# Block-sparse attention with a gated MLP on one core: q and k transposed by the whole array, and a new order of every queue

## The chip, the cores and the metric

The kernel runs on one core of a Trainium2 chip. The time is device time in microseconds (us) of one execution, the median over the runs shown. Five engines work side by side, each through its own queue in order: TensorE (PE; its weight loads are PEld), VectorE (DVE), ScalarE (ACT), GpSimd (POOL) and SyncE (SP), which here does nothing but issue DMAs.

## The reference

The input is q, k, v of shape (4 batches, 8 heads, 768 tokens, 64) and the weights of a gated MLP. Attention is causal and block-sparse: for each token the 6 best of 24 chunks of 32 keys are kept. A chunk's rank is an upper bound of the score, from the minimum and maximum of its keys.

```python
k_min = np.min(k_chunks, axis=3); k_max = np.max(k_chunks, axis=3)
ub = np.sum(np.maximum(q[..., None, :] * k_min[:, :, None], q[..., None, :] * k_max[:, :, None]), axis=-1)
ub = np.where(causal, ub, -1e9)
top_chunks = np.argsort(ub, axis=-1)[..., -6:]
scores = np.where(sel & causal_tokens, scale * q @ k.T, -1e9)
x = softmax(scores) @ v            # heads side by side: (batch, 768, 512)
h = gelu(x @ w_in); u, v = h[..., :512], h[..., 512:]
v_n = (v - mean) / sqrt(var + 1e-6) * g_ln
out = x + (u * (w_sg @ v_n + b_sg)) @ w_out
```

## The kernel before

**Work.** Two heads make a pair; there are 16 pairs, p = 0 to 15, four to a batch. For a pair, q and k come from memory token by token (128 tokens on the partitions, 6 groups of tokens, the two heads' 64 numbers side by side, tile `qn` or `kn`), are transposed on PE by `transposed`, lines 581 to 587 (matmul against the identity `identF`, line 567), and copied out of PSUM: q into `qT` (line 659), k of pairs 0 to 5 into `KA` (line 606), with the chunks' minimum and maximum taken from the same PSUM banks (line 596). For pairs 6 to 15 k is transposed by a DMA (line 623) and its minima come from line 613, so PE transposes 6 k's and 16 q's, 22 in all. The chunk bounds are the small matmuls of lines 696 (pairs 0 to 3) and 743; DVE picks the best six and makes a mask; scores are the matmuls of lines 852 and 858 (pairs 0 to 3, each head on 64 rows of the array) and 812 (pairs 4 to 15, the whole array); ACT takes the exponential (lines 873, 818); the product with v is lines 896 and 903, and line 919 scales it into `XS`.

**Transposing, as it is.** `tokens_T` (lines 561 to 570) issues 12 matmuls: for each of the 6 groups of tokens, the first 64 tokens on the upper half of the array's rows into one PSUM bank and the last 64 on the lower half into another (`tile_position=(64 * R, 0)`). The program counts the change between such row tiles and the whole array as a change of mode. Both banks are written by one entry of PE's queue, so both are given out at once, and bank R holds runs of 64 tokens that `half` (line 575) spreads over `qT` or `KA`.

**The MLP of a batch.** When the four pairs of a batch are in `XS`, it is transposed into `xT` (line 935 on PE for batch 0 and part of 3, otherwise by DMA, line 927). Then `moe_h`: six matmul groups for v (line 950), gelu (line 954), statistics (lines 959, 961, 963), the reciprocal root on POOL (line 965), its use (line 967), and the normalised `vhat` (line 978 on DVE, 973 on ACT); eight groups for u (line 990). `moe_g`: eight groups against w_sg (line 1007), each of which needs all of `vhat`; lines 1013 and 1017 on DVE; then the output product (line 1030), the residual into `osb` (line 1036, three buffers in turn), and the store (line 1043).

**Order.** All operations of the whole program are made once, as a list, and `TABLE` holds for each engine the numbers of that list in the order of its queue, the PSUM bank of each tile (`slots`) and the engine of those operations that can run on more than one (`engine`). Dependencies become semaphore waits by themselves; every queue is strictly in the order of its row. Five stages can be told apart on PE: start to batch 0's first line 950 (pairs 0 to 3), then from each batch's first line 950 to the next (attention of the next four pairs mixed with the MLP of this batch), and the last batch's MLP alone.

Of the kernel before, what the change touches and what calls it, by code (L numbers as in the profile page):

```python
# [249 lines left out]
def pe32(*cols):  # L250
    o = sum(c * 2 / 2.4 + 2.5 for c in cols) + 28
    return o, o + 136
# [6 lines left out]
def _build(nc, ctx, q, k, v, w_in, g_ln, w_sg, b_sg, w_out, out):  # L259
# [4 lines left out]
    NT = S // 128  # L264
    NC = S // 32
# [50 lines left out]
    RUN2 = 0  # L316
    FINE = (0,)
# [254 lines left out]
    def run(p):  # L572
        return 128 if p < RUN2 else 64

    def half(a, R, p):
        return a.rearrange("p (a R x) -> p R a x", R=2, x=run(p))[:, R]
# [4 lines left out]
    def transposed(p, nm, src, tag):  # L581
        s = p % NQS
        ts = [ps_g.tile() for _ in range(2)]
        P.op("pe", (pairs_T if p < RUN2 else tokens_T)(src[s], ts), (650, 820) if p < RUN2 else (412, 580), (tag, p),
             mode=3 if p < RUN2 else 1,
             reads=[(nm, s, i, h) for i in range(2) for h in range(2)] + ["identF"] + ["pewarm"] * (p == 0), writes=ts, alloc=tuple(ts))
        return ts

    def kside(p):
        w = p % NW  # L590
        ts = transposed(p, "kn", kn, "ktr")
        wv = lambda R, m: W[w][:, m, 0:NC].rearrange("p (a R c) -> p R a c", R=2, c=run(p) // 32)[:, R]
# [519 lines left out]
    for p in range(4, NP + 4):  # L1112
# [38 lines left out]
    "act": (  # L1151
# [10 lines left out]
    "dve": (  # L1162
# [105 lines left out]
```

How the kernel before makes its waits and increments, by code:

```python
        def run(e, eng):  # L186
            for i in self.order[e]:
                o = ops[i]
                need = {}
                for d in o.waits:
                    p = ops[d]
                    s = dsem[p.dma] if p.dma is not None else sems[p.eng]
                    key = p.dma if p.dma is not None else p.eng
                    if key not in need or need[key][1] < p.count:
                        need[key] = (s, p.count)
                for s, c in need.values():
                    eng.wait_ge(s, c)
                ins = o.fn(eng)
                if o.dma is not None:
                    ins.then_inc(dsem[o.dma], 16)
                elif o.inc:
                    ins.then_inc(sems[e], 1)
            if e == "sp":
                for d, idxs in self.dma_sems.items():
                    if ops[idxs[-1]].tag[0] == "st":
                        eng.wait_ge(dsem[d], 16 * len(idxs))
```

## Time and profile before

| | us |
|---|---|
| median of 3 runs | 216.65 |
| lowest, highest | 216.13, 218.79 |
| the profiled execution's own time | 217.55 |
| its span, first to last instruction | 215.4 |

The span lies inside the own time; 2.15 us lie around it. Times in rows count from the start of the span. Rows of a timeline give start, duration, engine, line, operation, what is written from what, shapes and count; in brackets the idle time of the engine just before and what ended it. A matmul's row includes its way through the array, so a matmul that follows at once starts before the row of the one ahead has ended; how long a group holds PE is read from its start to the start of the next.

### The profile page before, as it was taken

How to read it: one execution, taken by the hardware profiler on the slowest of the kernel's cores; microseconds unless marked ns; L12 is line 12 of the kernel's file. 1: busy time of each engine (PE TensorE's matmuls, PEld its weight loads, DVE VectorE, ACT ScalarE, POOL GpSimd, SP SyncE). 2: the span in 40 equal slices, each digit the busy share in tenths (PEclk: the TensorE clock that was granted, in tenths of full speed). 3: DMA queues.
4: the chain of work that ended last, by engine and by line, in shares of the span. 5: the costliest groups of instructions: out<-in, count | busy, mean ns of one | idle time of the engine just before them, and what ended most of it. 6: DMA issues, size and time to landing. Idle time of an engine off the chain costs nothing.

```text
span 215.4 us, 6383 instructions
## 1 busy us (share of the span) xinstructions
PE 194.8 (90%) x2549; PEld 126.0 (58%) x2564; DVE 185.5 (86%) x531; ACT 163.7 (76%) x247; POOL 132.8 (62%) x168
## 2 busy tenths in 40 slices
PE   7778897899999999997959989998995999999993
PEld 2445676745766577763535757873572677655652
DVE  3899999798999999969889999987779664888994
ACT  3559998799999999977795889979685698765010
POOL 5447699798799999994596795987059016002000
PEclk9999999999999999999999999999999799999999
DMA  7999999999998999999895838698500213103117
GB/s 147 218 221 252 213 214 336 227 270 257 198 235 189 229 203 215 200 171 195 177 219 117 190 76 203 130 173 203 104 3 2 53 35 88 49 0 127 70 49 243
DMA packets 96801, 35.02 MB, mean 163 GB/s; under 512 B 91514, under 2 KB 92292, under 8 KB 96772
## 3 DMA queue, kind: packets, MB, share of 16 engines
q1 hardware_dynamic: 95908, 33.70, 73.5%
q10 hardware_dynamic: 864, 0.92, 1.3%
q8 instruction: 20, 0.33, 0.7%
q14 instruction: 9, 0.07, 0.1%
HBM read 24.38 MB, written 6.29 MB: 142 GB/s over the span
## 4 chain that ended last, share of the span: by engine, by line
PE 44%; DVE 35%; ACT 11%; issue 3%; DMA 3%; POOL 2%; SPq 0%; DVEq 0%
PE PS L1007 8%; PE PS L950 8%; PE PS L812 7%; PE PS L1030 7%; DVE PS L1013 3%; DVE vhat L978 3%; PE PS L896 3%; DVE Bn L613 3%; DVE uT L1017 3%; PE PS L990 3%; DVE XS L919 3%; ACT vgb L954 2%; ACT E L873 2%; PE PS L696 2%; DVE KA L378 2%
## 5 line engine op out<-in xcount | busy, mean ns | idle before, releaser
L818 ACT ACTIVATE E<-PS 128x1024 bf16<-128x1024 f32 (+1 forms) x72 | 62.3, 924 | 9.2 <-PE PS L812 8.5
L1007 PE MATMUL PS<-wsgT,vhat 128*128 128x384 bf16 x192 | 35.9, 334 | 5.1 <-DVE vhat L978 4.7
L812 PE MATMUL PS<-QA,KA 128*128 128x128 bf16 (+2 forms) x336 | 36.1, 247 | 0.4 <-DVE rden L911 0.3
L812 PEld LDWEIGHTS PS<-QA,KA 128*128 128x128 bf16 x336 | 23.9, 98 | 10.9 <-ACT E L818 1.8
L823 POOL TENSOR_SCALAR_AFFINE_SELECT E<-E 128x768 bf16<-128x768 bf16 x24 | 20.4, 864 | 13.5 <-ACT E L818 12.8
L1007 PEld LDWEIGHTS PS<-wsgT,vhat 128*128 128x128 bf16 x192 | 18.3, 100 | 17.3 <-issue 6.2
L378 POOL CAST QA<-qT 64x768 bf16<-64x768 f32 (+1 forms) x27 | 22.2, 826 | 7.1 <-DVE qT L378 3.8
L995 ACT ACTIVATE uT<-PS 128x384 bf16<-128x384 f32 x32 | 15.1, 505 | 12.8 <-PE PS L990 12.7
L990 PE MATMUL PS<-xT,winb 128*128 128x384 bf16 x128 | 23.1, 326 | 0.0
L950 PE MATMUL PS<-winb,xT 128*128 128x512 bf16 x92 | 20.8, 379 | 2.4 <-issue 0.9
L873 ACT ACTIVATE E<-PS 128x1024 bf16<-128x1024 f32 (+1 forms) x24 | 20.5, 926 | 2.6 <-PE PS L858 2.4
L1030 PE MATMUL PS<-woutb,uT 128*128 128x512 bf16 (+1 forms) x98 | 21.8, 353 | 0.6 <-issue 0.2
L1013 DVE SCALAR_TENSOR_TENSOR PS<-PS,bgT,bsgbc 128x384 f32<-128x384 f32 x32 | 19.2, 614 | 2.3 <-PE PS L1007 2.3
L965 POOL TENSOR_TENSOR rstd<-rstd,neghalf 128x6 f32<-128x6 f32 x4 | 5.4, 1348 | 24.8 <-DVE rstd L963 24.8
L896 PE MATMUL PS<-vx,E 128*128 128x65 bf16 x480 | 19.3, 194 | 0.4 <-issue 0.4
L959 DVE BATCH_NORM_STATS2 stats<-vgb 128x6 f32<-128x512 f32 x24 | 16.0, 683 | 3.9 <-ACT vgb L954 3.8
L613 DVE TRANSPOSE_TENSOR_REDUCE Bn<-kn 128x24 f32<-128x768 f32 x20 | 18.9, 957 | 0.0
L1036 DVE TENSOR_TENSOR osb<-PS,XS 128x512 f32<-128x512 f32 x21 | 14.2, 681 | 4.9 <-PE PS L1030 3.2
L896 PEld LDWEIGHTS PS<-vx,E 128*128 128x128 bf16 x480 | 16.9, 98 | 2.0 <-issue 0.8
L1017 DVE TENSOR_TENSOR uT<-PS,uT 128x384 bf16<-128x384 f32 x32 | 17.4, 550 | 0.6 <-ACT uT L995 0.2
L990 PEld LDWEIGHTS PS<-xT,winb 128*128 128x128 bf16 x128 | 12.1, 98 | 8.6 <-ACT vgb L954 0.2
L919 DVE TENSOR_TENSOR XS<-PS,rden 128x384 bf16<-128x384 f32 x30 | 16.3, 550 | 0.5
(121 smaller groups left out, 388.3 us busy)
## 6 DMA issues: line engine op xcount, KB each, us to landing
qn<-in_q_dram SPq DMA_DIRECT2D x32, 192.0 KB, 5.2
vn<-in_v_dram SPq DMA_DIRECT2D x16, 384.0 KB, 5.3
out_dram<-osb SPq DMA_DIRECT2D x20, 256.0 KB, 2.6
kn<-in_k_dram SPq DMA_DIRECT2D x10, 384.0 KB, 5.9
kn<-in_k_dram SPq DMA_DIRECT2D x12, 192.0 KB, 4.5
uT<-in_moe_w_sg_dram SPq DMA_DIRECT2D x4, 384.0 KB, 5.9
vgb<-in_moe_w_in_dram SPq DMA_DIRECT2D x3, 512.0 KB, 7.7
vhat<-in_moe_w_sg_dram SPq DMA_DIRECT2D x2, 384.0 KB, 3.8
```

The costliest lines, as they stand in the source:

```text
L378: return e.tensor_copy(dst(), src())
L613: P.op("dve", lambda d, m=m, op=op: d.tensor_reduce(Bn[u][:, x, m, :], kn[s][:].rearrange("p i t d -> p (i t d)").rearrange("p (c x) -> p ...
L812: r = e.matmul(both(ts)[:, o:o + n], KA[w][i][:, 128 * kb:128 * kb + 128], QA[w][i][:, q0:q0 + n], start=True, stop=True)
L818: P.op("act", lambda e, ts=ts, c0=c0, c1=c1, i=i: e.activation(E[es][:, i, c0:c1], both(ts)[:, 0:c1 - c0], ACTF.Exp, scale=SCALE), act(c1 ...
L873: P.op("act", lambda e, ts=ts, c0=c0, c1=c1, n=n: e.activation(E[es][:, :, c0:c1], both(ts).rearrange("p (i x) -> p i x", i=2)[:, :, 0:n], ...
L896: r = e.matmul(t.ap()[:, 65 * qb:65 * qb + 65], E[es][:, i, a:a + 128], vx[w][:, kb, i, :], start=first, stop=False, skip_group_check=True)
L950: r = e.matmul(t.ap()[:, 0:F], xT[s][:, dk, 128 * qt:128 * qt + 128], winb[:, dk, F:DFF], start=(dk == 0), stop=(dk == NDK - 1))
L990: r = e.matmul(t.ap()[:, 0:TG], winb[:, dk, 128 * fb:128 * fb + 128], xT[s][:, dk, TG * tg:TG * tg + TG], start=(dk == 0), stop=(dk == NDK ...
L1007: r = e.matmul(t.ap()[:, 0:TG], vhat[s][:, sb, 128 * fb:128 * fb + 128], wsgT[:, sb, TG * tg:TG * tg + TG], start=(sb == 0), stop=(sb == N ...
L1013: P.op("dve", lambda d, t=t, fb=fb, tg=tg: d.scalar_tensor_tensor(t.ap()[:, 0:TG], t.ap()[:, 0:TG], bgT[:, NT + fb:NT + fb + 1], bsgbc[:, ...
L1017: P.op("dve", lambda d, t=t, fb=fb, tg=tg: d.tensor_tensor(gT[s][:, fb, TG * tg:TG * tg + TG], t.ap()[:, 0:TG], uT[s][:, fb, TG * tg:TG * ...
L1030: r = e.matmul(t.ap()[:, 0:c1 - c0], gT[s][:, fb, 128 * qt:128 * qt + 128], woutb[:, fb, c0:c1], start=(fb == 0), stop=(fb == NF - 1))
```

## The change

A pair with `p not in ROW64` (all, since `ROW64` is empty) is transposed by six matmuls on the whole array, 128 tokens by 128 numbers each. They are two entries of the queue with one bank each: the first three groups of tokens, and the last three. `half` and `wv` then address a contiguous half of the tokens.

```diff
+    ROW64 = ()
     def half(a, R, p):
+        if p >= RUN2 and p not in ROW64:
+            return a.rearrange("p (R a x) -> p R a x", R=2, x=run(p))[:, R]
         return a.rearrange("p (a R x) -> p R a x", R=2, x=run(p))[:, R]
     def transposed(p, nm, src, tag):
         s = p % NQS
         ts = [ps_g.tile() for _ in range(2)]
+        if p >= RUN2 and p not in ROW64:
+            rows = src[s][:].rearrange("p i t d -> p (i t d)")
+            for R, t in enumerate(ts):
+                def tr(e, R=R, t=t):
+                    for j in range(NT // 2):
+                        b = NT // 2 * R + j
+                        r = e.matmul(t.ap()[:, 128 * j:128 * j + 128], rows[:, 128 * b:128 * b + 128], identF[:], is_transpose=True)
+                    return r
+                P.op("pe", tr, pe32(*[128] * 3), (tag, p, R), reads=[...] + ["identF"] + ["pewarm"] * (p == 0), writes=[t], alloc=t)
+            return ts
         P.op("pe", (pairs_T if p < RUN2 else tokens_T)(src[s], ts), ...
-        wv = lambda R, m: W[w][:, m, 0:NC].rearrange("p (a R c) -> p R a c", R=2, c=run(p) // 32)[:, R]
+        wv = lambda R, m: W[w][:, m, 0:NC].rearrange("p (a R c) -> p R a c" if p < RUN2 or p in ROW64 else "p (R a c) -> p R a c", R=2, c=run(p) // 32)[:, R]
 TABLE = {
     "pe": (
-        "1 47 2 56 3 80 4 5 62 89 117 95 199 200 108 202 203 193 194 190 191 158 248 250 123 196 197 254 252 140 167 "
+        "1 47 48 2 3 57 58 82 83 64 93 92 4 5 123 122 99 201 202 207 213 113 208 214 112 198 199 204 205 165 129 210 "
...
```

All five rows of `TABLE`, the banks and the choice of engines are new. Lines of the changed kernel are 14 higher from the middle of the file on (line 1007 is 1021 there); the new transposes are its line 593. Counted from the tables, PE has 63 changes of mode before and 55 now (before and now): 28 and 35 up to batch 0's first line 950, 23 and 13 in the stage after it, 12 and 7 in the next. Between engines, some twenty small operations change places: for one, DVE now copies five halves of `qT` where it copied seven, and eight of the casts of later pairs' v and k go from POOL to ACT.

The first place is PE between batch 1's v groups (line 950, now 964) and the first product with w_sg (line 1007, now 1021), where line 1007 needs the whole of `vhat`. Before:

```order
L950 MATMUL PS<-winb,xT 128x512 x24
L990 MATMUL PS<-xT,winb 128x384 x28
L567 MATMUL PS<-identF,qn 128x64 x12
L990 MATMUL PS<-xT,winb 128x384 x4
L1007 MATMUL PS<-wsgT,vhat 128x384 x18
```

Now (line 1004 is the old 990, line 826 the old 812):

```order
L964 MATMUL PS<-winb,xT 128x512 x24
L1004 MATMUL PS<-xT,winb 128x384 x4
L593 MATMUL PS<-identF,qn 128x128 x3
L1004 MATMUL PS<-xT,winb 128x384 x8
L593 MATMUL PS<-identF,qn 128x128 x3
L1004 MATMUL PS<-xT,winb 128x384 x12
L593 MATMUL PS<-identF,qn 128x128 x3
L1004 MATMUL PS<-xT,winb 128x384 x8
L826 MATMUL PS<-QA_1,KA_1 128x384
L826 MATMUL PS<-QA_1,KA_1 128x128
L826 MATMUL PS<-QA_1,KA_1 128x384
L826 MATMUL PS<-QA_1,KA_1 128x128
```

Here one whole transpose of q stood among the u groups; now there are three half transposes, then a piece of the scores and a fourth half before line 1021.

The second place is SP's queue where batch 1's `XS` is transposed into `xT` by DMA (line 927, now 941), with the stores of batch 0's outputs (line 1043, now 1057) and loads around it. Before:

```order
L539 DMA kn<-in_k_dram 128x12x64 x2
L534 DMA qn<-in_q_dram 128x6x64
L927 DMA_TRANSPOSE xT<-XS 128x6x128
L1043 DMA out_dram<-osb 128x512
L927 DMA_TRANSPOSE xT<-XS 128x6x128 x3
```

Now:

```order
L1057 DMA out_dram<-osb 128x512 x3
L535 DMA qn<-in_q_dram 128x6x64 x2
L637 DMA_TRANSPOSE KA_0<-kbx 128x6x128
L540 DMA vn<-in_v_dram 128x12x64
L540 DMA kn<-in_k_dram 128x12x64
L941 DMA_TRANSPOSE xT<-XS 128x6x128 x4
```

The store that stood behind the first of the four transposes is now ahead of them all, together with two other stores.

The third place is DVE's queue from batch 1's variance (line 963, now 977) through the four parts of `vhat` (line 978, now 992). Before:

```order
L963 TENSOR_SCALAR rstd<-mv 128x6
L763 MAX m_1<-U 128x8 x9
L967 SCALAR_TENSOR_TENSOR nmr<-mv,rstd 128x6
L978 TENSOR_SCALAR vhat<-vgb,mv,rstd 128x512 x4
L768 TENSOR_TENSOR Dn<-U,m_1 128x576
```

Now:

```order
L977 TENSOR_SCALAR rstd<-mv 128x6
L627 TENSOR_REDUCE Bn<-kn 128x24
L777 MAX m_1<-U 128x8 x9
L981 SCALAR_TENSOR_TENSOR nmr<-mv,rstd 128x6
L992 TENSOR_SCALAR vhat<-vgb,mv,rstd 128x512 x2
L379 COPY qT<-PS 128x384
L992 TENSOR_SCALAR vhat<-vgb,mv,rstd 128x512 x2
```

A reduction of k now stands ahead of line 981, and a copy of half a `qT` between the second and the third part of `vhat`. In batch 2 the same stretch has five parts of `vhat` on DVE where it had four, and one of them left ACT.

## Rows read from the trace of the kernel before

**Rows 1.** Windows by stage: length; busy PE, PEld, DVE, ACT, POOL; PEclk, DMA, GB/s

```profile
0.00:15.00 15.00, 11.18 (x112) 5.06 (x113) 10.42 (x35) 6.88 (x12) 6.49 (x19) 1.00 1.13 192
15.00:44.10 29.10, 25.36 (x569) 19.03 (x568) 27.27 (x91) 25.71 (x33) 24.35 (x31) 1.00 1.07 243
44.10:99.40 55.30, 52.69 (x769) 34.68 (x775) 52.46 (x162) 51.93 (x82) 48.81 (x58) 1.00 1.07 217
99.40:149.30 49.90, 45.49 (x592) 29.87 (x595) 45.62 (x134) 41.55 (x59) 38.69 (x45) 1.00 0.78 166
149.30:186.20 36.90, 34.18 (x363) 22.77 (x365) 26.54 (x64) 28.50 (x49) 13.10 (x16) 0.95 0.24 55
186.20:215.40 29.20, 25.91 (x149) 14.59 (x150) 23.23 (x50) 9.15 (x17) 1.32 (x1) 1.00 0.27 94
```

**Rows 2.** Timeline of PE: its long waits after the first stage

```profile
97.53 0.59 PE L567 MATMUL PS<-identF,qn 64*128 64x64 f32 x12 [0.47 <-DVE osb L1036]
99.39 0.81 PE L950 MATMUL PS<-winb,xT 128*128 128x512 bf16 x3 [0.89 <-DMA xT<-XS]
...
112.71 3.08 PE L1007 MATMUL PS<-wsgT,vhat 128*128 128x384 bf16 x18 [2.37 <-DVE vhat L978]
...
126.61 0.72 PE L743 MATMUL PS<-qT,Wall 64*32 64x288 f32 x16 [0.82 <-DVE Wall L652]
...
149.31 1.02 PE L950 MATMUL PS<-winb,xT 128*128 128x512 bf16 x4 [0.92 <-issue]
...
164.17 1.14 PE L1007 MATMUL PS<-wsgT,vhat 128*128 128x384 bf16 x6 [2.32 <-DVE vhat L978]
165.78 1.98 PE L1007 MATMUL PS<-wsgT,vhat 128*128 128x384 bf16 x6 [0.29 <-DVE XS L919]
```

**Rows 3.** Timeline of PE: transposes of q and k (L567), whole-array f32 transposes (L511)

```profile
15.70 0.59 PE L567 MATMUL PS<-identF,kn 64*128 64x64 f32 x12
16.12 0.38 PE L852 MATMUL PS<-QA,KA 64*128 64x256 bf16 x4
...
51.97 0.81 PE L990 MATMUL PS<-xT,winb 128*128 128x384 bf16 x4
52.71 0.59 PE L567 MATMUL PS<-identF,qn 64*128 64x64 f32 x12
...
54.22 0.50 PE L491 MATMUL PS<-identB,XS 128*128 128x128 bf16 x6
54.56 1.46 PE L990 MATMUL PS<-xT,winb 128*128 128x384 bf16 x8
55.86 0.49 PE L511 MATMUL PS<-identF,bgT 128*128 128x128 f32 x3
56.19 0.50 PE L491 MATMUL PS<-identB,XS 128*128 128x128 bf16 x6
```

**Rows 4.** Timeline of SP's issues, and of DVE, before batch 1's line 950

```profile
92.81 0.36 SPq L1043 DMA_DIRECT2D out_dram<-osb  x1
93.22 4.35 SPq L927 DMA_TRANSPOSE xT<-XS  x3
...
96.79 0.69 DVE L1036 TENSOR_TENSOR osb<-PS,XS 128x512 f32<-128x512 f32 x1 [1.58 <-DMA out_dram<-osb]
```

**Rows 5.** Timeline of DVE: from the variance to vhat, batches 1 and 2

```profile
108.49 0.17 DVE L967 SCALAR_TENSOR_TENSOR nmr<-mv,rstd 128x6 f32<-128x6 f32 x1 [0.84 <-POOL rstd L965]
108.70 3.87 DVE L978 TENSOR_SCALAR vhat<-vgb,mv,rstd 128x512 bf16<-128x512 f32 x4
...
160.51 3.52 DVE L978 TENSOR_SCALAR vhat<-vgb,mv,rstd 128x512 bf16<-128x512 f32 x4
```

**Rows 6.** Groups by line and shape: count, busy us, mean ns, idle before

```profile
L613 DVE TRANSPOSE_TENSOR_REDUCE Bn<-kn 128x24 f32<-128x768 f32 x20 | 18.9, 957 | 0.0
L995 ACT ACTIVATE uT<-PS 128x384 bf16<-128x384 f32 x32 | 15.1, 505 | 12.8 <-PE PS L990 12.7
L375 ACT ACTIVATE qT<-PS 128x384 f32<-128x384 f32 x25 | 11.2, 509 | 3.0 <-PE PS L567 2.9
```

More of the change, by code:

```diff
@@ L583, in transposed @@
         ts = [ps_g.tile() for _ in range(2)]
+        if p >= RUN2 and p not in ROW64:
[6 more added lines that the diff above has]
+                    return r
+                P.op("pe", tr, pe32(*[128] * 3), (tag, p, R), reads=[(nm, s, i, h) for i in range(2) for h in range(2)] + ["identF"] +
+                     ["pewarm"] * (p == 0), writes=[t], alloc=t)
+            return ts
         P.op("pe", (pairs_T if p < RUN2 else tokens_T)(src[s], ts), (650, 820) if p < RUN2 else (412, 580), (tag, p),
@@ L1136 @@
     "pe": (
[14 rows of a table removed]
-    "act": (
[10 rows of a table removed]
-    "dve": (
[16 rows of a table removed]
-    "pool": (
[12 rows of a table removed]
-    "slots": (
-        "7314540635701767417545434327664501450123017623544450145016745767215354160145450101237305501452301450141"
-        "3253136406153734136267206061520463145674567016732310123452345454774213567016723450104250167014523675763"
-        "4121051765072355610147332155450467672345454554370167016723234216644167010123230123066767010167451752414"
-        "3511004157267361266727074160101676723234301234523674575454523452367750012301014501435654023273353454272"
-        "4540161502447"),
-    "engine": (
[10 rows of a table removed]
[14 rows of a table added]
+    "act": (
[10 rows of a table added]
+    "dve": (
[16 rows of a table added]
+    "pool": (
[12 rows of a table added]
+    "slots": (
+        "7561032056760167461232440100044545230145232323332454567236745453675124576767010101452703601670145450104"
+        "7523124162630752161763605765332426667456767454517600123454545016604372345230145010176674501450145012104"
+        "4501543051513352000021654315365767670101232322750145014567452367054701670167456732336723010123231027325"
+        "7205152675603335223254450274501454567674201670101236724670167010145231676745456745742736321636471020523"
+        "3176640732602"),
+    "engine": (
[11 rows of a table added]
 }
```

121 rows, old and new, of the table TABLE are left out of this document.

## The prediction

> **What bounds the kernel now.** I read the windows by stage first, because the work between the stages differs too much for one share of the whole span. A row there gives the stretch, its length, and the busy time of PE, PEld, DVE, ACT and POOL. In the first two rows [rows 1] DVE is the fullest from 15 us on: 27.27 of 29.10 us, PE 25.36, ACT 25.71. From 44.1 to 99.4 four engines are full at once: PE is idle for 2.6 us, DVE for 2.8, ACT for 3.4. From 99.4 to 149.3 all have some air (PE 4.4 us idle, DVE 4.3). From 149.3 PE leads, and the last 29.2 us are the last batch's MLP. So no single engine is the bound, and work that is taken off one engine is worth nothing unless a wait closes with it.
>
> The second view is PE's timeline with its idle time in brackets. After 44.1 us PE's idle time lies in a few places [rows 2]: 0.47 and 0.89 us before batch 1's line 950, 2.37 before its line 1007, 0.82 before a chunk-bound matmul, 0.92 before batch 2's line 950, 2.32 and 0.29 in batch 2's line 1007. The reader is to see that most of them end with a DVE or a DMA result, not with a matmul. After the 2.32 us PE's clock is lower: six matmuls that take 1.14 us at 164.17 take 1.98 at 165.78, and the stage's mean granted clock is 0.95 [rows 1, 2], between the levels of 2.4 and 1.2 GHz; 5% of 36.9 us is 1.8 us. After the 2.37 us of batch 1 it stayed at 1.00 [rows 1].
>
> **The transposes themselves.** A transpose holds PE from its start to the next group's start. Between neighbours that use row tiles too it is 16.12 - 15.70 = 0.42 us [rows 3]. Whole-array f32 transposes of 128 by 128 stand in the trace already, at line 511: three of them hold PE for 56.19 - 55.86 = 0.33 us, so the new six cost 0.66, that is 0.24 more. For 22 transposes this is +5.3 us of PE. The ends of this price: if three of them held PE for their whole row of 0.49, it would be 0.98 - 0.42 = +0.56 each, +12.3 in all; and the price can go below nothing where the neighbours use the whole array, since a change of mode also costs. Four matmuls of line 990 hold PE for 0.65 (55.86 - 54.56 for eight), but 52.71 - 51.97 = 0.74 when a row-tiled transpose follows: 0.09 for a change of mode [rows 3]. A transpose with whole-array neighbours so loses two of them, 0.18. I take 0.24 and 0.09, the nearest rows, and count the changes by the tables: 63 to 55, -0.7 us.
>
> The Trainium skill ("TensorEngine Tiling (Array Packing)", Key Properties) says that changing the tiling mode drains TensorE. Rows 3 show a part of that alone, 0.09 us a change. An estimate from a full drain, the 0.16 us by which the row of line 990 outlasts its hold, would make the saving 8 x 0.16 = 1.3 us in place of 0.7; I keep the measured one.
>
> The copies out of PSUM now address contiguous halves. A copy of 384 numbers on ACT takes 509 ns into spread runs (line 375) and 505 into a contiguous one (line 995) [rows 6]: nothing to gain or lose.
>
> **Start to 44.1 us.** Twelve transposes: 12 x 0.24 = +2.9; seven more changes of mode, 7 x 0.09 = +0.6; two transposes of w_sg (line 491) that come into this stage, 54.56 - 54.22 = 0.34 each, +0.7 [rows 3]. That is +4.2 us of PE. What hides it is PE's idle time here, 3.8 us before 15 us and 3.7 after [rows 1]. Five of the twelve transposes lie in the first stretch, where PE waits for loads and minima; about 3.0 of the 4.2 fall in the second, where 3.7 are idle and DVE stays the fuller engine. If the cover is gone, all 4.2 show; if it holds, none. PE would then be busy for 28.4 of 29.1 us beside a DVE that is busy for 27.3, and two queues this full seldom fit without loss. I take +0.5.
>
> **44.1 to 99.4 us.** PE's work: seven transposes +1.7, ten changes of mode fewer -0.9, two transposes of w_sg gone -0.7; +0.1. The wait at the end closes: today the store issued at 92.81 stands in SP's queue behind the first DMA transpose and ahead of the other three [rows 4]; DVE waits 1.58 us for it to free `osb` [rows 4], PE 0.47 for DVE, and then 0.89 for the last transpose, which went out at the end of the 4.35 us that three issues take [rows 2, 4]. In the new order the three stores are ahead, so 0.47 and 0.89 go, -1.36. What is late next is DVE: two copies of `qT` (0.51 each by ACT's row) and one reduction of a k (0.96) come into its queue here while other work leaves [rows 6]; of some +1 us net I charge +0.4, as the 1.58 us wait leaves room. Sum -0.9.
>
> **99.4 to 149.3 us.** The 2.37 us wait ends with `vhat`. Between batch 1's last line 950 and its first line 1007 PE gets four half transposes of 0.33 for one whole of 0.52 (+0.8), and a piece of the scores of 1024 columns, 0.65 x 1024/1536 = 0.4. On DVE's side the reduction of 0.96 goes into an idle 0.84 [rows 5, 6], and a `qT` copy of 0.51 stands between parts of `vhat`: 0.6 later. The wait shrinks by 0.8 + 0.4 - 0.6 = 0.6. The 0.82 us wait gets five groups of work in front where two stand now, and I take 0.6 off. For the 0.92 us I see nothing that removes it: a store still stands between the DMA transposes. PE's work: three transposes +0.7, five changes fewer -0.45, one product with v (`pv`, line 896) that comes in from the next stage +0.45: +0.7. Sum -0.5.
>
> **149.3 to 186.2 us.** DVE makes five parts of `vhat`, not four, at 3.52/4 = 0.88 [rows 5]; the work that fills PE's wait is the same within 0.2 us, so the 2.32 us wait becomes about 3.2; the product with v that left gives back 0.45. Sum +0.5, with the same fall of the clock.
>
> **186.2 us to the end.** The same groups, PE and DVE in the same lengths: 0.
>
> **The sum.** +0.5 - 0.9 - 0.5 + 0.5 = -0.4 us on the profiled execution's own 217.55, so 217.15; the median of the runs shown is 0.9 below that execution, so 216.2. By about 2% (4.3 us) a measurement of this kernel can tell a difference from none; -0.4 is none.
>
> **Rivals.** *Slower: PE becomes the bound of the first stage.* The place is 15 to 44.1 us, the price what of +4.2 finds no idle PE; it decides once more than half of the 3.7 us [rows 1] is idle that can't be filled, because PE there waits for exponentials to free its banks. Then +3.5 to +4.2 in place of +0.5: 219.7. For it: half transposes stand between row-tiled scores, with two changes of mode each. Against it: DVE's work there, which sets the pace today, doesn't grow.
>
> *Faster: the waits close.* All of rows 2 are 8.1 us, and the lower clock 1.8 more; if half of the 9.9 goes beside the work that is added, 216.65 - 4.9 = 211.7. For it: the waits end at a few named places, and every queue has been laid anew. Against it: the stage at 149.3 looks worse, not better, and the engines left are full.
>
> *The array is held longer.* If each group of three held PE for its whole 0.49, PE would have +12.3, of which perhaps 4 find idle time: 225. The Trainium skill speaks for something like it ("TensorE: Matmul & The Clock Gate", Part 4: PE-mode transpose): it gives about 275 ns for a 128 by 128 bf16 transpose inside a kernel. By its figure, an estimate, six in a row would take 1.65 us if nothing overlapped. Rows 3 show three f32 ones in 0.33, so they do overlap.
>
> That the new way is no different in copies and chunk minima is already in the sum.
>
> **How the numbers follow.** The forecast, near 216.2 and good for 214.2 to 218.2, gets 0.48; the waits closing 0.25; PE as the bound 0.22; the longer hold 0.05. Faster by over 2% (under 212.3): 0.6 of the waits' case, 0.15, and 0.02 from the forecast's edge, 0.17. Slower by over 2% (over 221.0): a third of PE's case, 0.08, most of the longer hold, 0.04, and 0.02, together 0.14. Within: 0.69. The range of 211.0 to 220.8 leaves out a third of the waits' case and about as much of the two slow ones, 0.2 in all.
>
> **What would show it.** Right: line 593's groups of three start 0.33 us apart; batch 0's first line 950 starts between 43.5 and 45.5; no idle time from a store before batch 1's line 950; about 1.8 us idle before its line 1007, and about 3 in batch 2; the last batch's MLP takes 29 us. Wrong: the first stage ends at 47 or later with PE idle for less than 5 us in it, or batch 2's wait is under 1.5 us with the clock at 1.00, or the groups of three start 0.45 apart.

## The result and the profile after

| | before | after |
|---|---|---|
| median (lowest to highest), run side by side, 4 executions each | 216.43 us (216.13 to 218.79) | 209.38 us (209.12 to 212.02) |
| the profiled execution: own time, span | 217.55, 215.4 | 209.12, 207.4 |

The ratio after to before is 0.968 (95% interval 0.958 to 0.978): faster by 3.2%. A ratio leaves disturbed executions out and a median does not, so a ratio below can differ from the quotient of the medians beside it. The forecast was 216.2 with a range of 211.0 to 220.8, so the result lies below the range. Line numbers of the changed kernel are 14 higher than before in the parts spoken of here: 950 is now 964, 978 is 992, 1007 is 1021, 965 is 979; the new transposes are line 593.

The windows by stage of the changed kernel, cut at the first line 964 of each batch, come first; the columns are those of [rows 1].

```profile
0.00:15.00 15.00, 13.06 (x103) 7.04 (x104) 10.87 (x39) 6.13 (x12) 9.98 (x23) 1.00 1.13 193
15.00:43.48 28.48, 27.14 (x519) 20.02 (x518) 26.21 (x91) 26.05 (x38) 21.84 (x28) 1.00 1.09 263
43.48:99.10 55.62, 52.52 (x720) 35.85 (x721) 53.65 (x162) 52.05 (x78) 50.91 (x62) 1.00 1.14 214
99.10:146.32 47.22, 46.19 (x594) 31.58 (x594) 42.27 (x141) 42.41 (x61) 32.77 (x40) 1.00 0.96 179
146.32:178.01 31.69, 31.69 (x349) 21.29 (x350) 22.75 (x53) 28.54 (x49) 10.20 (x12) 1.00 0.22 59
178.01:207.40 29.39, 26.22 (x153) 14.55 (x152) 23.66 (x50) 9.30 (x17) 1.32 (x1) 0.99 0.23 81
```

Set against [rows 1], the fourth stage is 2.7 us shorter (49.90 to 47.22) and the fifth 5.2 (36.90 to 31.69): 7.9 of the 8.0 us. The other four rows add up to nearly nothing. The clock of the fifth stage is 1.00 where it was 0.95. In that stage PE is busy without a break.

PE's timeline of the changed kernel, at the places of [rows 2]:

```profile
99.10 1.67 PE L964 MATMUL PS<-winb,xT 128*128 128x512 bf16 x7 [2.78 <-DMA xT<-XS]
...
111.16 0.50 PE L593 MATMUL PS<-identF,qn 128*128 128x128 f32 x3
111.50 2.11 PE L1021 MATMUL PS<-wsgT,vhat 128*128 128x384 bf16 x12
...
146.32 1.02 PE L964 MATMUL PS<-winb,xT 128*128 128x512 bf16 x4 [0.95 <-DMA xT<-XS]
...
159.05 3.09 PE L1021 MATMUL PS<-wsgT,vhat 128*128 128x384 bf16 x18
```

The two waits of 2.37 and 2.32 us for `vhat` are gone: line 1021 starts at 111.50 and 159.05 right behind other matmuls, with no bracket. The waits for the DMA transposes in front of a batch's MLP are not gone: 0.95 us in front of batch 2's, as before, and 2.78 in front of batch 1's, where it was 0.89.

What became of the wait for `vhat` stands in DVE's timeline of the changed kernel, to be laid beside [rows 5]:

```profile
109.02 1.00 DVE L992 TENSOR_SCALAR vhat<-vgb,mv,rstd 128x512 bf16<-128x512 f32 x2
...
110.40 0.99 DVE L992 TENSOR_SCALAR vhat<-vgb,mv,rstd 128x512 bf16<-128x512 f32 x2
...
154.59 0.20 DVE L977 TENSOR_SCALAR rstd<-mv 128x6 f32<-128x6 f32 x1
...
156.25 0.17 DVE L981 SCALAR_TENSOR_TENSOR nmr<-mv,rstd 128x6 f32<-128x6 f32 x1 [1.47 <-POOL rstd L979]
156.46 2.37 DVE L992 TENSOR_SCALAR vhat<-vgb,mv,rstd 128x512 bf16<-128x512 f32 x5
```

Five parts of batch 2 take 2.37 us here; four took 3.52 [rows 5]. The instruction is the same, with the same shape. So the duration does not belong to the instruction alone. The row of a line with its durations (least, median and greatest, in ns, of 16) says it for the kernel before:

```profile
L978 DVE TENSOR_SCALAR vhat<-vgb,mv,rstd x16: 535/880/1085, 56.9 to 196.9; 128x512 bf16<-128x512 f32 x16
```

and for the changed kernel:

```profile
L992 DVE TENSOR_SCALAR vhat<-vgb,mv,rstd x16: 536/542/889, 56.2 to 188.9; 128x512 bf16<-128x512 f32 x16
```

The least is the same, 0.54 us; the median fell from 0.88 to 0.54. What stood beside the long ones is in POOL's timeline of the kernel before, in batch 2:

```profile
158.28 1.35 POOL L965 TENSOR_TENSOR rstd<-rstd,neghalf 128x6 f32<-128x6 f32 x1 [8.63 <-DVE rstd L963]
159.59 0.86 POOL L823 TENSOR_SCALAR_AFFINE_SELECT E<-E 128x768 bf16<-128x768 bf16 x1
160.52 1.46 POOL L378 COPY QA<-Dt 32x576 bf16<-32x576 bf16 x2
162.04 0.90 POOL L378 CAST QA<-qT 64x768 bf16<-64x768 f32 x1
163.01 0.74 POOL L378 COPY QA<-Dt 32x576 bf16<-32x576 bf16 x1
```

and in the changed kernel:

```profile
154.87 1.34 POOL L979 TENSOR_TENSOR rstd<-rstd,neghalf 128x6 f32<-128x6 f32 x1
162.91 0.86 POOL L837 TENSOR_SCALAR_AFFINE_SELECT E<-E 128x768 bf16<-128x768 bf16 x1 [6.69 <-ACT E L832]
```

Before, POOL idled for 8.63 us ahead of the reciprocal root and then ran five instructions back to back while DVE made `vhat`. DVE's last two `vhat` of that batch, taken one by one from the kernel before:

```profile
162.18 1.04 DVE L978 TENSOR_SCALAR vhat<-vgb,mv,rstd 128x512 bf16<-128x512 f32 x1
163.15 0.88 DVE L978 TENSOR_SCALAR vhat<-vgb,mv,rstd 128x512 bf16<-128x512 f32 x1
```

The first ends at 163.22, 0.28 us behind POOL's cast (162.04 + 0.90 = 162.94); the second ends at 164.03, 0.28 us behind POOL's copy (163.01 + 0.74 = 163.75). The other two of this batch and the four of batch 1 end 0.28 us behind a POOL instruction as well. In the new order the idle time lies behind the root: POOL does nothing for 6.69 us, and `vhat` is made in 2.37.

### The profile page after: what moved, and what is told of

Its sections match the earlier page's. It is cut to its first block, busy times and chain, and to the rows that moved or that the text cites. A ratio compares the mean times of both kernels' runs of the same rounds, so it can differ in the third digit from the quotient of the medians.

```text
span 207.4 us, 6132 instructions
## 1 busy us (share of the span) xinstructions
PE 196.8 (95%) x2432; PEld 130.3 (63%) x2432; DVE 179.4 (87%) x532; ACT 164.5 (79%) x251; POOL 127.0 (61%) x163
## 4 chain that ended last, share of the span: by engine, by line
PE 74%; DMA 10%; DVE 8%; ACT 3%; SPq 3%; issue 2%; DVEq 0%
PE PS L1021 15%; PE PS L826 12%; PE PS L1044 8%; PE PS L964 8%; PE PS L1004 8%; DMA kn<-in_k_dram 6%; PE PS L910 6%; PE PS L593 5%; DMA xT<-XS 3%; PE PS L917 3%; ACT E L887 2%; PE PS L757 2%; PE PS L866 2%; PE PS L710 2%; DVE Bn L627 2%
## 5 line engine op out<-in xcount | busy, mean ns | idle before, releaser
L1021 PE MATMUL PS<-wsgT,vhat 128*128 128x384 bf16 x192 | 34.5, 326 | 0.3 <-DVE wsgT L379 0.3
L964 PE MATMUL PS<-winb,xT 128*128 128x512 bf16 x96 | 22.0, 379 | 4.8 <-DMA xT<-XS 3.7
L1044 PE MATMUL PS<-woutb,uT 128*128 128x512 bf16 (+1 forms) x108 | 23.8, 355 | 0.0
L1004 PE MATMUL PS<-xT,winb 128*128 128x384 bf16 x128 | 23.6, 326 | 0.0
L964 PEld LDWEIGHTS PS<-winb,xT 128*128 128x128 bf16 x96 | 9.0, 98 | 15.6 <-issue 3.3
L968 ACT ACTIVATE vgb<-PS 128x512 f32<-128x512 f32 x24 | 13.8, 595 | 6.3 <-PE PS L964 6.1
L1031 DVE TENSOR_TENSOR uT<-PS,uT 128x384 bf16<-128x384 f32 x32 | 16.8, 547 | 0.4
```

What stands on the lines that cost most here:

```text
L964: r = e.matmul(t.ap()[:, 0:F], xT[s][:, dk, 128 * qt:128 * qt + 128], winb[:, dk, F:DFF], start=(dk == 0), stop=(dk == NDK - 1))
L1004: r = e.matmul(t.ap()[:, 0:TG], winb[:, dk, 128 * fb:128 * fb + 128], xT[s][:, dk, TG * tg:TG * tg + TG], start=(dk == 0), stop=(dk == NDK ...
L1021: r = e.matmul(t.ap()[:, 0:TG], vhat[s][:, sb, 128 * fb:128 * fb + 128], wsgT[:, sb, TG * tg:TG * tg + TG], start=(sb == 0), stop=(sb == N ...
L1044: r = e.matmul(t.ap()[:, 0:c1 - c0], gT[s][:, fb, 128 * qt:128 * qt + 128], woutb[:, fb, c0:c1], start=(fb == 0), stop=(fb == NF - 1))
```

## The experiments

Three theories were set against each other. **P**: a `vhat` on DVE is held up by the POOL instruction beside it, and the new order leaves POOL idle there. **O**: DVE's chain simply starts earlier against PE's work, and POOL plays no part. **T**: the whole-array transposes bring the gain. Later runs add one on the DMA transposes, **D**: a transpose is late because transfers that SP issued just ahead of it are still moving; and its rival, **X**: its input is late, or its issue takes long for its own sake. Medians are over 4 executions of each kernel; runs 1, 4, 6 and 7 were taken beside the kernel before at 217.49 us, runs 5, 8, 9 and 11 beside it at 217.55, runs 2, 3 and 10 beside it at 216.40.

**1. The kernel before, POOL's queue alone changed.** The numbers are those of the list of operations: 736 and 1007 are the reciprocal roots of batches 1 and 2; the others are POOL's casts, copies and mask selects. Operations 547 and 977 also wait for DVE's last `vhat` (741, 1013).

```diff
-  736 644 815 547
+  644 815 736 547
-  1007 1079 977 978 931 980 932 1102 966 960
+  1079 931 966 960 932 1007 977 978 980 1102
         P.place(order, slots)
+        for o, d in ((547, 741), (977, 1013)):
+            P.ops[o].deps.add(d)
```

> The kernel before, with POOL's queue alone changed: in batch 1 and batch 2 the casts and mask selects that POOL ran while DVE made vhat stand ahead of the reciprocal root (line 967's producer) or wait until DVE's last vhat is done. Theory P (a vhat on DVE is stretched by the POOL instruction beside it): each vhat of batches 1 and 2 takes 0.54 us, not 0.88 to 1.09; DVE's vhat of batch 2 end near 161.8 in place of 164.0; PE's waits of 2.37 and 2.32 before line 1007 shrink to under 0.6 each, the clock stays at 1.00 after the second; 210 to 212.5 us in all. Theory O (DVE's chain simply starts earlier against PE's work in the new order, POOL plays no part): vhat stay at 0.88 or more each, and the time stays at 215.5 to 217.5. Theory T (the whole-array transposes bring the gain): also 215.5 to 217.5.

Measured: 210.96 us (210.02 to 211.98) against 217.49 before, ratio 0.980 (0.968 to 0.993). Run once more beside others (run 3), the same kernel took 210.77 against 216.40, ratio 0.971 (0.962 to 0.981). Both intervals lie below 1, so there is a gain; neither lies wholly below 0.98, so a gain of over 2% is not certain. DVE's timeline around batch 2's `vhat`, then POOL's, then PE's in both batches:

```profile
155.40 0.17 DVE L963 TENSOR_SCALAR rstd<-mv 128x6 f32<-128x6 f32 x1
...
157.24 1.91 DVE L978 TENSOR_SCALAR vhat<-vgb,mv,rstd 128x512 bf16<-128x512 f32 x4
```

```profile
155.66 1.35 POOL L965 TENSOR_TENSOR rstd<-rstd,neghalf 128x6 f32<-128x6 f32 x1 [2.39 <-DVE rstd L963]
159.22 2.29 POOL L378 COPY QA<-Dt 32x576 bf16<-32x576 bf16 x3 [2.21 <-DVE vhat L978]
```

```profile
110.39 1.46 PE L1007 MATMUL PS<-wsgT,vhat 128*128 128x384 bf16 x8 [0.42 <-DVE vhat L978]
...
159.30 1.14 PE L1007 MATMUL PS<-wsgT,vhat 128*128 128x384 bf16 x6
...
160.46 1.14 PE L1007 MATMUL PS<-wsgT,vhat 128*128 128x384 bf16 x6
...
163.84 1.04 PE L812 MATMUL PS<-QA,KA 128*128 128x128 bf16 x11
```

Its fourth and fifth stage, from the windows:

```profile
98.81:146.69 47.88, 45.72 (x598) 30.04 (x597) 43.52 (x135) 42.64 (x61) 38.94 (x45) 1.00 0.83 172
146.69:179.19 32.50, 32.41 (x363) 21.83 (x364) 24.02 (x64) 28.19 (x49) 13.38 (x16) 1.00 0.26 60
```

Four `vhat` take 1.91 us in place of 3.52, with no change to the order of DVE, PE, ACT or SP. PE's wait falls from 2.37 to 0.42 us in batch 1 and is gone in batch 2. The stages are 2.0 and 4.4 us shorter than in [rows 1]; the span is 208.6, 6.8 less than before, out of the 8.0 that the whole change brought. The stage ahead of these two, which the edit does not touch, is 1.1 us shorter as well; in runs 2 and 3 it is 0.6 and 1.4 shorter, so that part is a difference between executions and not the edit's. DVE's and PE's orders are the old ones, and so are the transposes: O and T cannot give this.

**2. The kernel before, batch 2's part of that edit alone.** The first pair of lines and the wait of 547 are left out of the diff above.

> The kernel before with POOL's queue changed around batch 2's vhat alone; batch 1 as it was. Theory P: the stage from batch 2's first line 950 to batch 3's (36.9 us before) takes 32 to 33 us, with no wait over 0.5 us before line 1007 and the clock at 1.00, the stage in front of it stays at 49 to 50 us with the wait of 2.4 us; 212 to 213.5 us in all, some 2 us above the kernel with both batches' queues changed. Theory O (DVE's earlier start counts, not POOL): no gain beyond 1 us.

Measured: 214.42 us (212.41 to 215.38), ratio 0.988 (0.980 to 0.996). The windows of the fourth and fifth stage:

```profile
98.79:148.37 49.58, 45.89 (x596) 30.01 (x597) 45.27 (x134) 41.22 (x59) 38.13 (x44) 1.00 0.80 170
148.37:180.85 32.48, 32.40 (x364) 21.81 (x364) 24.48 (x64) 28.61 (x49) 13.94 (x17) 1.00 0.24 58
```

The stage with the edit is 4.4 us shorter, the one without it keeps its length, and its wait of 2.37 us:

```profile
112.33 1.46 PE L1007 MATMUL PS<-wsgT,vhat 128*128 128x384 bf16 x8 [2.37 <-DVE vhat L978]
```

The median is higher than expected: the profiled execution took 212.41 at a mean clock of 0.999, the other three 214.38 to 215.38 at 0.990 to 0.992, so the clock fell somewhere in them. No trace shows where; the one long wait for `vhat` that is left is batch 1's.

**3. Both parts again, beside run 2.**

> The kernel before with POOL's queue changed around the vhat of batches 1 and 2, as in the first run, beside the kernel with batch 2's alone. Theory P: 210 to 211.5 us, 2 us below the other, the difference in the stage from batch 1's first line 950 to batch 2's.

Measured: 210.77 us (210.34 to 213.68). The fourth stage took 48.24 us, 1.3 less than in run 2, though 1.31 us of waiting for the DMA transposes came back at its end. The medians of the two kernels lie 3.65 us apart where 2 were expected, the spans of the profiled executions 1.5 (210.3 and 208.8).

**4. The changed kernel, POOL made busy beside `vhat`.** Five casts into memory that nothing reads, right behind batch 2's reciprocal root (operation 1029).

```diff
+    spare = U[0][0:64].rearrange("p b c -> p (b c)").bitcast(BF16)[:, 0:S]
+    for n in range(5):
+        P.op("pool", lambda g: g.tensor_copy(spare, bsgbc[0:64, :]), gps(S), ("spare", n),
+             reads=[("bsgbc", 0), ("bsgbc", 1)], writes=["spare"])
+        P.ops[-1].deps.add(998)
...
+        i = order["pool"].index(1029) + 1
+        order["pool"][i:i] = range(len(P.ops) - 5, len(P.ops))
```

> The changed kernel, with five more casts of 64 by 768 on POOL (into memory that nothing reads any more) right behind the reciprocal root of batch 2, where POOL is idle for 6.7 us. All else is the same, and the output too. Theory P: the five vhat of batch 2 on DVE take 0.85 to 1.05 us each in place of 0.54, the last ends near 160.6 in place of 158.83, PE waits 1 to 2 us before its first line 1021 of batch 2, and the time is 1 to 3.5 us longer (the upper end if PE's clock falls too): 210.5 to 213. Theories O and T: POOL's casts lie beside other work, the time stays within 0.5 us of 209.4.

Measured: 213.61 us (211.06 to 215.53). DVE's, POOL's and PE's timelines at the place:

```profile
158.23 0.77 DVE L981 SCALAR_TENSOR_TENSOR nmr<-mv,rstd 128x6 f32<-128x6 f32 x1 [1.47 <-POOL rstd L979]
159.04 4.44 DVE L992 TENSOR_SCALAR vhat<-vgb,mv,rstd 128x512 bf16<-128x512 f32 x5
```

```profile
158.16 4.58 POOL L1148 CAST U<-bsgbc 64x768 bf16<-64x768 f32 x5
```

```profile
163.62 4.71 PE L1021 MATMUL PS<-wsgT,vhat 128*128 128x384 bf16 x18 [2.44 <-DVE rden L925]
```

`vhat` takes 4.44 us in place of 2.37, and PE waits 2.44 us where it had not waited at all. The bracket names the reciprocal behind `vhat`, but it is the end of `vhat`, at 163.48, that came late. Four of the five `vhat` end 0.28 us behind one of the casts. Even the small line 981, on 6 numbers, takes 0.77 in place of 0.17. And the 18 matmuls after the wait take 4.71 us; in the changed kernel they took 3.09. The window over them has the granted clock, 0.64, between the levels of 1.2 and 2.4 GHz:

```profile
163.62:168.20 4.58, 4.58 (x19) 2.30 (x20) 2.74 (x6) 1.43 (x2) 1.64 (x2) 0.64 0.00 0
```

The direction is P's; the wait and the time lie above P's 1 to 2 us and 210.5 to 213.

**5. The same five casts, held back until `vhat` is done.** The control: the same work on POOL, one place later.

```diff
         P.place(order, slots)
+        P.ops[-5].deps.add(1036)
```

> The changed kernel with the same five extra casts on POOL as in the run that put them beside DVE's vhat of batch 2, but held back until DVE's last vhat of that batch is done, so that they lie beside copies and products that read PSUM. Theory P (only the DVE instructions that are held up by a POOL instruction count): vhat at 0.54 us each, PE without a wait at line 1021, the time within 0.7 us of the changed kernel's. Rival (POOL's extra work costs time wherever it stands, for instance by delaying the mask selects behind it on its queue): 2 us longer or more, as with the casts beside vhat.

Measured: 210.04 us (208.44 to 212.16), with the changed kernel itself at 209.97 beside it. The timelines of DVE, POOL and PE again:

```profile
155.62 2.37 DVE L992 TENSOR_SCALAR vhat<-vgb,mv,rstd 128x512 bf16<-128x512 f32 x5
```

```profile
158.05 4.36 POOL L1148 CAST U<-bsgbc 64x768 bf16<-64x768 f32 x5 [2.67 <-DVE vhat L992]
```

```profile
158.21 3.09 PE L1021 MATMUL PS<-wsgT,vhat 128*128 128x384 bf16 x18
```

The casts cost nothing here that these runs can tell, 0.07 us by the medians. It is not POOL's load that counts but what DVE does beside it.

**6. The whole-array transposes alone, in the old order.**

```diff
-        P.op("pe", (pairs_T if p < RUN2 else tokens_T)(src[s], ts), (650, 820) if p < RUN2 else (412, 580), (tag, p),
-             mode=3 if p < RUN2 else 1,
+        rows = src[s][:].rearrange("p i t d -> p (i t d)")
+        def tr(e):
+            for b in range(NT):
+                r = e.matmul(ts[b // 3].ap()[:, 128 * (b % 3):128 * (b % 3) + 128], rows[:, 128 * b:128 * b + 128], identF[:], is_transpose=True)
+            return r
+        P.op("pe", tr, pe32(*[128] * 6), (tag, p),
...
-        return a.rearrange("p (a R x) -> p R a x", R=2, x=run(p))[:, R]
+        return a.rearrange("p (R a x) -> p R a x", R=2, x=run(p))[:, R]
```

> The kernel before with its own order of all queues, but each of the 22 transposes made by six matmuls of the whole array, three into each of the same two banks, and the copies and minima on contiguous halves. Theories P and O: PE gets 22 x 0.24 = 5.3 us more, less 0.09 us for each change of mode that goes; part of it lies beside waits; 217 to 220 us, with the waits of 2.3 us before line 1007 still there. Theory T: the time falls by 2 us or more, to under 214.5.

Measured: 217.65 us (217.28 to 218.19) against a median of 217.49, ratio 1.012 (1.0005 to 1.0225). The line of busy times on the page, and PE's waits:

```profile
PE 199.4 (92%) x2432; PEld 130.9 (61%) x2432; DVE 186.3 (86%) x531; ACT 164.2 (76%) x247; POOL 132.9 (61%) x168
```

```profile
113.33 0.97 PE L1012 MATMUL PS<-wsgT,vhat 128*128 128x384 bf16 x5 [2.35 <-DVE vhat L983]
...
166.35 1.14 PE L1012 MATMUL PS<-wsgT,vhat 128*128 128x384 bf16 x6 [2.33 <-DVE vhat L983]
```

PE is busy for 4.6 us more than before, and the span is 216.1, 0.7 more. T falls: the transposes bring nothing by themselves, and cost little: 0.2 us by the medians, about 1% by the ratio.

**7. Row tiles again, in the new order.** 14 of the 22 transposes are written as before the change; both banks are filled by the entry that comes first (for q of pair 5 two places later), and the other one is empty. The other eight stay whole.

```diff
-    ROW64 = ()
+    ROW64 = (0, 1, 2, 5, 6, 7, 8, 9, 10, 11)
...
+        n, line = len(P.ops), TABLE["pe"].split()
+        late = line.index(str(n)) > line.index(str(n + 1))
+        if late:
+            P.op("pe", lambda e: None, (0, 0), (tag, p, 0))
+        P.op("pe", tokens_T(src[s], ts), (412, 580), (tag, p, int(late)), mode=1,
...
+        if not late:
+            P.op("pe", lambda e: None, (0, 0), (tag, p, 1))
```

> The changed kernel with its own order of all queues, but 14 of the 22 transposes (k of pairs 0, 1, 2, 5; q of pairs 0 to 2 and 5 to 11) made by row tiles again, at the place of the earlier of their two halves; for the other eight the order uses the two banks one after the other, so they stay. Theories P and O: PE is relieved of 14 x 0.24 = 3.4 us, less what the changes of mode cost; the time is 206.5 to 209.5. Theory T: the time rises by 14/22 of what the change brought, some 4 us, to 212 or more.

Measured: 211.00 us (209.87 to 213.42), above what P and O expected and below T's figure. The PE time that was to be saved does not show: the wait before batch 2's line 964 is 2.04 us where the changed kernel has 0.95. Together with run 6: 4.6 us of PE's time added by the kind of transpose, or 1.4 taken away (PE is busy for 195.4 us here and for 196.8 in the changed kernel), hardly reach the end.

**8. The changed kernel once more**, as the measure for runs 5, 9 and 11.

> The changed kernel itself once more, unaltered, beside the others on one chip. All theories: 209 to 210 us, PE idle for 2.5 to 3 us before batch 1's first line 964 and about 1 us before batch 2's.

Measured: 209.97 us (209.38 to 211.50), ratio 0.967 (0.959 to 0.975). The wait before batch 1's MLP was 2.05 us this time, not 2.5 to 3. In runs 4, 5 and 7, which have the same order on SP, it was 2.65, 1.09 and 2.40.

**9. The changed kernel, SP's queue altered.** 435 is the load of v of pair 8; 567, 628, 667 and 728 are batch 1's four DMA transposes; 858, 955 and 1003 three of batch 2's; 819 is a store.

```diff
-  592 435 690 567 628 667 728 726
+  592 690 567 628 667 728 435 726
-  919 917 857 792 954 798 795 979 943 858 819 955 1003 813
+  919 858 917 857 792 954 798 795 979 943 955 1003 819 813
```

> The changed kernel with SP's queue alone altered: in front of batch 1's MLP the load of v of pair 8 (384 KB) goes behind the four DMA transposes instead of ahead of them; in front of batch 2's the first transpose goes out eight places earlier, and one store (of osb) behind the last transpose. Theory D (the first transpose is issued slowly, 4.17 us against 1.28 for its neighbours, because the loads just ahead of it are still moving): its issue takes under 2.7 us, PE's idle time before batch 1's first line 964 falls from 2.78 to under 1.5 us and before batch 2's from 0.95 to under 0.3; 1.5 to 2.8 us less than the changed kernel. Rival X (what is late are the attention outputs, or a transpose's issue takes long for its own sake): both waits stay within 0.5 us of what they were, the time too.

Measured: 208.86 us (208.31 to 209.57), 1.1 below the changed kernel beside it, where D gave 1.5 to 2.8. It has the lowest median of this study, but its ratio to the kernel before, 0.960 (0.954 to 0.966), and that of run 8, 0.967 (0.959 to 0.975), overlap. SP's issues in the changed kernel of the first profile,

```profile
87.79 0.57 SPq L540 DMA_DIRECT2D vn<-in_v_dram  x1
88.48 0.76 SPq L540 DMA_DIRECT2D kn<-in_k_dram  x1
89.29 8.16 SPq L941 DMA_TRANSPOSE xT<-XS  x4
```

and in this one:

```profile
87.51 0.51 SPq L540 DMA_DIRECT2D kn<-in_k_dram  x1
88.08 6.33 SPq L941 DMA_TRANSPOSE xT<-XS  x4
```

PE's two waits in this run:

```profile
96.70 2.54 PE L964 MATMUL PS<-winb,xT 128*128 128x512 bf16 x11 [0.16 <-issue]
...
145.39 0.81 PE L964 MATMUL PS<-winb,xT 128*128 128x512 bf16 x3 [1.58 <-DVE Dn L782]
```

Batch 1's part does what D says: the four issues end at 94.41 in place of 97.45, the first of them took 1.58 us in place of 4.17, and the wait is gone. The evidence is not clean, though: runs 10 and 11 have the same order here, and in them the first issue took 1.76 and 3.05 us and the wait was 0.36 and 1.05; run 5, with the old order, had 2.39 and 1.09. Batch 2's part does not do what D says: the wait is 1.58 us, longer than before. The bracket there names DVE, whose instruction ended at 145.27; the last of that batch's transposes landed at 145.30, 0.09 us ahead of PE's start, as it did in the changed kernel (146.23, with PE's start at 146.32).

**10. One more move on SP: the transpose of k of pair 14 behind batch 2's last two.**

```diff
-  979 943 955 1003 819 813 918
+  979 955 1003 943 819 813 918
```

> The run with SP's queue altered in front of batches 1 and 2, with one more move: the DMA transpose of k of pair 14 goes behind the last two transposes of batch 2's attention output, not ahead of them. In that run those two were issued as soon as their inputs were there, at 138.89 and 140.48, but landed 3.7 and 4.8 us after their issue began, with PE idle for 1.58 us. Theory D (what is still moving makes a transpose late): they land about a microsecond sooner, PE's idle time before batch 2's first line 964 is 0.3 to 1.0 us, 207.5 to 208.6 us in all. Rival X (their inputs come too late): 1.4 us or more stay, and the time as well.

Measured: 209.56 us (207.11 to 210.63), and PE waits 1.70 us. This is X's figure for the wait; with this spread the time tells nothing. What makes batch 2's transposes late stays open.

**11. Row tiles for the 14 and SP's queue altered, together.**

> The changed kernel with 14 of its 22 transposes on row tiles again (PE busy for 195.4 us in place of 196.8 when this was run alone, but idle 2.0 us before batch 2's first line 964) and with SP's queue altered as in the run above. If the waits on the DMA transposes were what kept the saved PE time from showing: 206 to 207.5 us, below both the changed kernel and the run with SP's queue alone. If other engines set the pace between the waits: no faster than the run with SP's queue alone.

Measured: 209.20 us (208.10 to 211.69), no faster than run 9. Other engines set the pace between the waits.

## Why the prediction was wrong, point by point

The table gives each stage's change against [rows 1] in us: the forecast, the change itself, POOL's queue alone (run 1) and the transposes alone (run 6).

| stage | forecast | measured | POOL alone | transposes alone |
|---|---|---|---|---|
| start to batch 0's MLP | +0.5 | -0.6 | +0.5 | +1.1 |
| to batch 1's | -0.9 | +0.3 | -1.1 | -0.8 |
| to batch 2's | -0.5 | -2.7 | -2.0 | +1.8 |
| to batch 3's | +0.5 | -5.2 | -4.4 | -1.7 |
| last MLP | 0 | +0.2 | +0.2 | +0.2 |
| sum | -0.4 | -8.0 | -6.8 | +0.7 |

(In run 6 the clock fell behind batch 1's wait and not behind batch 2's, hence +1.8 and -1.7.)

**The step that failed** is in the stage from 149.3 us: "DVE makes five parts of `vhat`, not four, at 3.52/4 = 0.88 [rows 5]", and so the wait of 2.32 us was to become "about 3.2", "with the same fall of the clock". Five parts took 2.37 us, 0.54 each with an overlap of 0.08. The 0.88 was measured correctly, but beside POOL's casts, and I carried it into an order in which POOL is idle there. The prediction read DVE's row and never POOL's beside it. A second sign lay in the same trace: the least of the 16 durations was 0.535 us.

Worked again with what the runs showed, and with two more rows of the kernel before:

```profile
158.02 0.17 DVE L963 TENSOR_SCALAR rstd<-mv 128x6 f32<-128x6 f32 x1
...
170.84 1.04 PE L812 MATMUL PS<-QA,KA 128*128 128x128 bf16 x11
```

In the kernel before, the variance ended at 158.19 and the last `vhat` on DVE at 164.03, 5.84 us later; PE had work until 161.86, 3.67 us of it, and the rest of 2.2 is the wait. In the changed kernel the same way takes 158.83 - 154.79 = 4.04 us, with one part more, and PE has work until 159.05, 4.26 us. So DVE's side shrank by 1.8, and PE's work behind the variance grew by 0.6, where the prediction had it "the same within 0.2 us". The second alone would have left 5.84 - 4.26 = 1.6 us of waiting, the first alone 4.04 - 3.67 = 0.4. Run 1, which has the old fill and four parts, had 159.16 - 155.57 = 3.59 against 3.67, and no wait.

**The fall of the clock** followed from the same error. Taken by PE's rows, the way from the matmul at 165.78 to the one at 170.84 cost 5.06 us before; in run 1 the same way, from 160.46 to 163.84, cost 3.38. With the wait gone the stage has a clock of 1.00 in the changed kernel and in runs 1 to 3. Wait and clock together make the 4.4 us of run 2. The prediction had all of them in view (2.32 + 0.29 + 1.8), and left them where they were.

**The stage from 99.4 us** failed by the same price: its wait was to shrink by 0.6 of 2.37 and vanished. The 0.82 us before a chunk-bound matmul went as well, as it was said in part (0.6). The 0.92 us before batch 2's MLP stayed, as forecast: 0.95.

**The stage from 44.1 us**: the waits that a store caused are gone, as forecast, but the gain of 1.36 us is not there. What is late next is not DVE, as the prediction had it, but the DMA transposes themselves: the first was issued right behind two loads of 384 KB and took 4.17 us to issue, its three neighbours 1.28 each. In run 9 one of the loads stands behind the transposes, and the wait, 1.1 to 2.8 us in five traces of the other order, is gone; since run 11 kept 1.05 us of it, how much of the wait is the loads' is not settled.

**The transposes** were priced nearly right. Three of them hold PE for 111.50 - 111.16 = 0.34 us (forecast 0.33). In front of row-tiled scores a group of three holds PE longer: one that starts at 15.64 in the changed kernel has the scores' matmuls start at 16.12, 0.48 us later, that is 0.15 for the change of mode, where 0.09 was taken. In the first stage PE is busy for 40.20 us in place of 36.54, 3.7 more (forecast +4.2), and as the stage is no longer for it, all of it went beside idle time. Run 6 adds 4.6 us of PE for all 22, 0.21 each (forecast +0.24), and 0.7 of that reaches the end of the span. Batch 0's MLP starts at 43.48, just under "between 43.5 and 45.5", and the last MLP takes 29.4 us, as said.

**The rivals.** "The waits close" was the one that came true, at 0.25; its 211.7 was too high since it counted half of the waits and the clock. What it lacked was a mechanism, and so its chance stayed small. "PE becomes the bound of the first stage" did not come: that stage is 0.6 us shorter. "The array is held longer" is ruled out by the 0.34; its sign, groups 0.45 apart, shows beside changes of mode alone.

Of the 8.0 us run 1, with POOL's queue alone changed, gives 6.8, and 6.4 of them lie in the two stages of its edit. What makes the rest stays open: the new order of DVE and PE was not tried alone.

## What to carry to other kernels

A duration from a trace belongs to the instruction and to what ran beside it: before pricing a moved DVE instruction by its row, read the least and the median of its line, and where they differ, read POOL's timeline over the long ones. When PE waits for a short chain of DVE instructions from SBUF to SBUF, keep POOL's casts, copies and mask selects out of just that chain, ahead of it or held back behind it; here that alone, without moving one instruction of any other engine, was worth 5.6 and 6.5 us of 217 by the medians of two comparisons (ratios 0.971 and 0.980). A large rewrite of the order is best read stage by stage, and the most conspicuous edit in the diff need not be the one that pays.

## What the runs showed of the hardware that was not expected

**DVE and POOL hold each other up.** A `vhat` of 0.54 us alone becomes 0.88 to 1.09 beside POOL's instructions, and a line on 6 numbers 0.77 in place of 0.17; nothing in the profile marks this as a wait, since it lies inside DVE's busy time. POOL pays less: five casts take 4.58 us beside `vhat` (run 4) and 4.36 behind it (run 5). All eight `vhat` of the kernel before's batches 1 and 2 on DVE end 0.28 us after a POOL instruction, whether that one took 0.74 or 1.01 us. Such a fixed distance speaks for waiting until that one is finished, and not for sharing. The Trainium skill says so ("SBUF — State Buffer", Who interferes with whom): DVE and GpSimd share a pair of SBUF ports under an exclusive lock, and when a DVE instruction runs in a mode that uses these ports too, the one of the two that comes second is blocked for the other's whole instruction; `tensor_scalar`, the kind that makes `vhat`, is among those that the page says can enter such a mode. The rows of runs 4 and 5 agree with it: 4.44 us beside five casts, 2.37 without them. In which mode `vhat` ran, no row shows.

**The clock after a wait differs from execution to execution.** In run 4, whose traced execution has the wait of 2.4 us, one of four executions kept a mean clock of 1.000 and took 211.06 us; the other three had 0.992 and took 213.52 to 215.53. So the same program runs with the fall of TensorE's clock and without it. They differ by 2.5 us or more there, but only one of the four was traced, so how much of this is the clock is not shown; of the kernel before beside run 2, the execution at 1.000 took 215.64 us and others at 0.992 took 215.90 to 217.03. One fall is priced by rows: 5.06 us against 3.38 for the same matmuls. In [rows 1] it fell behind batch 2's wait (0.95), in run 6 behind batch 1's (0.97 in that stage, 1.00 in the next).

**The first of four DMA transposes can take three times as long to issue as the next**: 4.17 us against 1.28, right behind two loads of 384 KB. Over five traces of this order it took 2.39 to 4.24 us, and 1.58 to 3.05 in runs 9 to 11, with one of the two loads moved behind. That the loads are the cause is likely from this, and not shown.
